# Tile 0 of a two-MLP kernel: half-width elementwise steps, bank-by-bank waits, and weight remainders split by groups on GpSimd

## What is computed

```python
w = exp(weight - max(weight)); w = w / (sum(w) + 1e-9)
x = sum over k of w[head, k] * x_pad[:, s + k, :]       # (2, 4096, 192)
x = x.reshape(8192, 192)
h = x @ w_in1;  g = h * clip(h + 3, 0, 6) / 6;  x = g @ w_out1      # 192 -> 2048 -> 192
h = x @ w_in2;  g = where(h > 0, h, exp(min(h, 0)) - 1)
out = g @ w_out2
```

## Time and profile before

| | us |
|---|---|
| median of 3 executions | 1120.57 (1120.43 to 1121.04) |
| profiled execution, its own time | 1120.58 |
| its span | 1118.7 |
| PE busy | 1113.0 (99% of the span), 9736 matmuls |
| DVE busy | 901.3 |
| ACT busy | 633.6 |
| POOL busy | 39.2, 36 instructions |

### The profile page before, as it was taken

One profiled execution on the slowest core, in us unless ns is written; L12 is line 12 of the kernel. 1 busy time (PEld: TensorE's weight loads), 2 busy tenths in 40 slices (PEclk: granted clock), 3 DMA queues, 4 the chain that ended last, 5 costly groups with the idle time before them and its releaser, 6 DMA issues.

```text
span 1118.7 us, 24069 instructions
## 1 busy us (share of the span) xinstructions
PE 1113.0 (99%) x9736; PEld 1014.5 (91%) x9736; DVE 901.3 (81%) x964; ACT 633.6 (57%) x685; POOL 39.2 (4%) x36
## 2 busy tenths in 40 slices
PE   9999999999999999999999999999999999999998
PEld 7999999999999999999999999999999999999997
DVE  8897887878888788787878878788787887876776
ACT  7765646556555554655555555465555655546544
POOL 3422000000000000000000000000000000000000
PEclk9999999999999999999999999999999999999999
DMA  4310010100101001010010100001000010000000
GB/s 158 117 59 10 1 34 0 33 0 0 33 0 33 0 0 33 0 33 0 0 33 0 33 0 1 32 0 33 0 24 9 0 33 0 9 5 11 6 2 29
DMA packets 10664, 22.48 MB, mean 20 GB/s; under 512 B 1424, under 2 KB 1424, under 8 KB 10640
## 3 DMA queue, kind: packets, MB, share of 16 engines
q1 hardware_dynamic: 10496, 22.12, 6.1%
q10 hardware_dynamic: 144, 0.01, 0.0%
HBM read 15.83 MB, written 6.29 MB: 20 GB/s over the span
## 4 chain that ended last, share of the span: by engine, by line
PE 98%; DVE 1%; DMA 0%; issue 0%; ACT 0%; DVEq 0%
PE h_ps L695 31%; PE acc_a L709 31%; PE acc_b L717 21%; PE h_ps L702 15%; DVE conv_a L466 0%; DMA taps<-tap_w 0%; PE h_ps L725 0%; DVE hidden L528 0%; PE acc_a L783 0%; PE acc_a L757 0%; PE acc_b L765 0%; PE acc_b L759 0%; PE acc_b L777 0%; PE acc_a L764 0%; PE acc_a L758 0%
## 5 line engine op out<-in xcount | busy, mean ns | idle before, releaser
L353 ACT CAST g_hi<-hidden 128x1024 fp32r<-128x1024 f32 x255 | 268.8, 1054 | 351.7 <-DVE hidden L533 238.2
L537 DVE TENSOR_TENSOR g_lo<-hidden,g_hi 128x1024 fp32r<-128x1024 f32 x255 | 312.9, 1227 | 127.7 <-ACT g_hi L353 127.7
L695 PE MATMUL h_ps<-in_hi_a,win_hi_a 64*128 64x512 f32 x1012 | 390.7, 386 | 0.0
L709 PE MATMUL acc_a<-g_hi,wout_hi_a 64*128 64x512 f32 x1012 | 390.7, 386 | 0.0
L695 PE MATMUL h_ps<-in_hi_a,win_lo_a 64*128 64x512 f32 x1012 | 390.6, 386 | 0.0
L709 PE MATMUL acc_a<-g_hi,wout_lo_a 64*128 64x512 f32 x1012 | 390.6, 386 | 0.0
L695 PE MATMUL h_ps<-in_lo_a,win_hi_a 64*128 64x512 f32 x1012 | 390.6, 386 | 0.0
L717 PE MATMUL acc_b<-g_hi,wout_b 64*128 64x512 f32 x1012 | 350.3, 386 | 0.0
L709 PE MATMUL acc_a<-g_lo,wout_hi_a 64*128 64x512 f32 x1012 | 310.1, 386 | 0.0
L717 PE MATMUL acc_b<-g_lo,wout_b 64*128 64x512 f32 x1012 | 310.0, 386 | 0.0
L528 DVE SCALAR_TENSOR_TENSOR hidden<-hidden,h_ps 128x1024 f32<-128x1024 f32 x128 | 156.3, 1221 | 59.0 <-ACT hidden L343 58.8
(11 more groups left out here) (112 smaller groups left out, 1212.9 us busy)
## 6 DMA issues: line engine op xcount, KB each, us to landing
xwin_a<-x_win SPq DMA_DIRECT2D x16, 259.0 KB, 2.8
raw_in<-w_in SPq DMA_DIRECT2D x8, 512.0 KB, 3.6
out_t<-out_a SPq DMA_DIRECT2D x16, 256.0 KB, 2.9
xwin_b<-x_win SPq DMA_DIRECT2D x15, 259.0 KB, 2.9
raw_out<-w_out SPq DMA_DIRECT2D x8, 384.0 KB, 3.9
out_t<-out_b SPq DMA_DIRECT2D x16, 128.0 KB, 2.3
xnext_b<-x_win SPq DMA_DIRECT2D x1, 259.0 KB, 5.5
taps<-tap_w ACTq DMA_DIRECT2D x1, 7.0 KB, 2.6
```

What stands on the lines that cost most here:

```text
L353: nc.scalar.copy(g_hi[:, g % PARTS, :], hidden[:, g % 2, :]).then_inc(hi_ready, 1)
L537: nc.vector.tensor_tensor(g_lo[:, g % PARTS, :], hidden[:, g % 2, :], g_hi[:, g % PARTS, :].bitcast(F32), ALU.subtract).then_inc(lo_ready, 1)
L695: return nc.tensor.matmul(bank(g, c), w[HALVES[r], columns(g, c)], x[HALVES[r], :], start=start, stop=c == 0 and r == 1 and term == 2)
L709: return nc.tensor.matmul(acc_a[acc][:, :], w[HALVES[r], g * CPG + c, :], x[HALVES[r], g % PARTS, c * TOK:(c + 1) * TOK], start=g == 0 and ...
```

## The change

1. ACT makes the relu of groups 0 and 1 in two halves, one for each bank; the first signals the new `act_half`, the second `act_done`.
2. DVE multiplies these two groups in halves (`nonlinear_halves`), with the new `g_half` after the first and `g_ready` after the second. Tap 0 goes ahead of group 0, and the finish of the b rows of tile 1 between groups 0 and 1.
3. `first_product` (group 2) waits before bank 0 for `g_half` and before bank 1 for `g_ready`.
4. ACT now makes the high parts of groups 0 and 1 back to back, then casts the a half of piece 3, then the relu of group 2, then casts the b half of piece 3.
5. POOL makes the low parts of pieces 2 and 3 in parts of one group each. `w_split` then counts: 1 is `win_lo_b` of piece 1 (waits for `act_half` 1); 2 and 3 are `wout_lo_a` and `wout_b` of group 0 (`act_half` 2); 4 is `win_lo_a` of group 4, 5 is `wout_lo_a` of group 1, 6 is `win_lo_b` of group 4, 7 is `wout_b` of group 1, 8 and 9 are `win_lo_a` and `win_lo_b` of group 5 (all wait for `act_done` 3, the relu of group 2). 10 and 11 are piece 4 as before, `wout_lo_a` and `wout_b` of groups 2 and 3.
6. PE waits for the parts of its group, and SP for the last part of a piece, before the buffer is filled again.

```diff
+        SPLITS = ([(1, 1, None), (2, 0, 0), (2, 1, 0), (3, 0, 0), (2, 0, 1), (3, 1, 0), (2, 1, 1), (3, 0, 1), (3, 1, 1)]
+                  + [(n, half, None) for n in range(4, ALL_PIECES) for half in range(2)])
+        BY_GROUPS = (2, 3)
+
+        def split(eng, n, half, part=1):
...
-                eng.wait_ge(w_split, h - 2)
+                eng.wait_ge(w_split, SPLITS.index((n, half, part if n in BY_GROUPS else None)) + 1)
...
-            together = [0, 0, 0, 0, 0, 1, 1, 2, 3, 3, 4, 4, 5, 5, 6, 7]
-            for n in range(1, ALL_PIECES):
+            together = {4: (3, 3), 5: (4, 4), 6: (5, 5), 7: (6, 7)}
+            for n, half, part in SPLITS:
+                raw, hi, lo = piece_views(n)[half]
+                if part is not None:
+                    if piece(n)[1] == 0:
+                        c = slice(part * CPG * P, (part + 1) * CPG * P)
+                        raw, hi, lo = raw[:, c], hi[:, c], lo[:, c]
+                    else:
+                        c = slice(part * CPG, (part + 1) * CPG)
+                        raw, hi, lo = raw[:, c, :], hi[:, c, :], lo[:, c, :]
+                h = 2 * n + half
                 piece_loaded(pool, n)
...
+                pool.wait_ge(w_hi, h + 1)
+                if n == 1 or (n == 2 and part == 0):
+                    pool.wait_ge(act_half, n)
+                elif n in BY_GROUPS:
+                    pool.wait_ge(act_done, 3)
+                else:
+                    pool.wait_ge(act_done, (together[n][half] if n < 8 else max(h - 9, GROUPS)) + 1)
+                nc.gpsimd.tensor_tensor(lo, raw, hi.bitcast(F32), ALU.subtract).then_inc(w_split, 1)
...
-            nonlinear(0, 0, 0)
-            nonlinear(0, 0, 1)
+            for g in range(2):
+                act.wait_ge(h_ready, g + 1)
+                for c, done in enumerate((act_half, act_done)):
+                    cols = slice(c * TOK, (c + 1) * TOK)
+                    nc.scalar.activation(hidden[:, g, cols], h_ps[g][:, cols], ACT.Relu,
+                                         bias=three[:, 0:1]).then_inc(done, 1)
             high_part(0, 0)
-            high_weights(3)
             high_part(0, 1)
+            piece_loaded(act, 3)
+            for half, (raw, hi, lo) in enumerate(piece_views(3)):
+                if half == 1:
+                    nonlinear(0, 0, 2)
+                nc.scalar.copy(hi, raw).then_inc(w_hi, 1)
             for g in range(2, GROUPS):
-                nonlinear(0, 0, g)
+                if g > 2:
+                    nonlinear(0, 0, g)
...
+            def nonlinear_halves(g):
+                for c in range(CPG):
+                    v = hidden[:, g, c * TOK:(c + 1) * TOK]
+                    dve.wait_ge((act_half, act_done)[c], g + 1)
+                    nc.vector.scalar_tensor_tensor(out=v, in0=v, scalar=6.0, in1=h_ps[g][:, c * TOK:(c + 1) * TOK],
+                                                   op0=ALU.min, op1=ALU.mult).then_inc((g_half, g_ready)[c], 1)
...
+            dve.wait_ge(tap_chain, 5)
+            conv_tap_a(0)
+            nonlinear_halves(0)
             dve.wait_ge(rest_done, 2)
             nc.vector.scalar_tensor_tensor(out=conv_b[:, :], in0=xnext_b[:, TAPS - 1:TAPS - 1 + TOK],
...
-            dve.wait_ge(tap_chain, 5)
-
-            nonlinear(0, 0, 0)
-            conv_tap_a(0)
-            nonlinear(0, 0, 1)
+            nonlinear_halves(1)
...
             def in_weights(m, g, load, half):
-                if load and g % 2 == 0:
-                    split(pe, number(m, 0, g // 2), half)
+                if load and (g % 2 == 0 or number(m, 0, g // 2) in BY_GROUPS):
+                    split(pe, number(m, 0, g // 2), half, g % 2)
...
                 in_weights(m, g, load, 0)
-                pe.wait_ge(g_ready, base + g - 1)
                 for c in range(CPG):
+                    pe.wait_ge((g_half, g_ready)[c], base + g - 1)
                     in_whole(m, g, src, c)
```

More of the change, by code:

```diff
@@ L144, in build @@
         act_done = sem("act_done")
+        act_half = sem("act_half")
+        g_half = sem("g_half")
         expm1_done = sem("expm1_done")
@@ L186, in number @@
             return 2 * PIECES * m + ORDER.index((kind, k))
-        def split(eng, n, half):
+        SPLITS = ([(1, 1, None), (2, 0, 0), (2, 1, 0), (3, 0, 0), (2, 0, 1), (3, 1, 0), (2, 1, 1), (3, 0, 1), (3, 1, 1)]
+                  + [(n, half, None) for n in range(4, ALL_PIECES) for half in range(2)])
+        BY_GROUPS = (2, 3)
+        def split(eng, n, half, part=1):
             h = 2 * n + half
@@ L289, in _ @@
                                         channel_multiplier=1).then_inc(ident_set, 1)
-            together = [0, 0, 0, 0, 0, 1, 1, 2, 3, 3, 4, 4, 5, 5, 6, 7]
-            for n in range(1, ALL_PIECES):
-                piece_loaded(pool, n)
[L295 to L301, removed]
+            together = {4: (3, 3), 5: (4, 4), 6: (5, 5), 7: (6, 7)}
[9 more added lines that the diff above has]
+                h = 2 * n + half
+                piece_loaded(pool, n)
+                pool.wait_ge(w_hi, h + 1)
[6 more added lines that the diff above has]
+                nc.gpsimd.tensor_tensor(lo, raw, hi.bitcast(F32), ALU.subtract).then_inc(w_split, 1)
         @block.scalar
@@ L734, in in_weights @@
             def in_weights(m, g, load, half):
-                if load and g % 2 == 0:
-                    split(pe, number(m, 0, g // 2), half)
+                if load and (g % 2 == 0 or number(m, 0, g // 2) in BY_GROUPS):
+                    split(pe, number(m, 0, g // 2), half, g % 2)
             def out_weights(m, g, load, half):
-                if load and g % 2 == 0:
-                    split(pe, number(m, 1, g // 2), half)
+                if load and (g % 2 == 0 or number(m, 1, g // 2) in BY_GROUPS):
+                    split(pe, number(m, 1, g // 2), half, g % 2)
             def first_product(m, base, g, src, load):
                 in_weights(m, g, load, 0)
-                pe.wait_ge(g_ready, base + g - 1)
                 for c in range(CPG):
+                    pe.wait_ge((g_half, g_ready)[c], base + g - 1)
                     in_whole(m, g, src, c)
@@ L939, in _ @@
             pair(1, "first")
-            pe.wait_ge(w_split, 2 * ALL_PIECES - 3)
+            pe.wait_ge(w_split, len(SPLITS))
             with nc.Fori(2, TILES - 1, engines=[mybir.EngineType.PE], hint_back_edge=True) as i:
```

## The result

The changed kernel has a median of 1122.39 us (1121.94 to 1123.42, 22 runs), the kernel before 1120.82 beside it (1120.36 to 1121.50, 22 runs). The ratio is 1.0015, with a 95% interval of 1.0009 to 1.0021: slower by 1.57 us, less than the 0.2% (2.24 us) by which the chances were set, but clear of noise with so many runs. The profiled execution took 1121.98 us, its span is 1120.2.

A forecast was written before the change was run, and what follows sets the result against it. PE's entry into its gapless stretch at 26.40 was taken to bound the kernel; -0.13 + 0.57 + 0.17 + 0.34 = +0.95 on 1120.58 gave 1121.5 us, range 1120.2 to 1122.6.

The forecast's parts named there:

- What bounds the kernel: PE is busy without gaps from 26.40 to 1107.00, so only its entry into that stretch moves the total.
- The gain: Tile 0: low part of group 0 ends at 18.40 instead of 18.53, so PE gains 0.13 us (bounds 0 to 0.25).
- (a): PE's first matmul of group 2, at 15.33, waited for DVE and could start at 14.85: 0.48 us lost.
- Turns of POOL and DVE: DVE steps with two SBUF operands and POOL remainders exclude each other and alternate, first asker first; low part 1.09 after release.
- Losses of rounds 4 and 5: PE waits for POOL's late count 7 (0.57), count 10 (0.17) and count 11 (0.34 us).
- the restarts: PE restarting after a stall can cost 0.07 more each, a bound of up to +1.2 us in total.
- The tie: POOL's count 9 at 24.44 against DVE's tap 2 at 24.50, given to POOL, ending at 25.18.
- rival 1: The near tie at 24.5 goes to DVE, PE starts round 5 at 28.2: +1.8, 1122.4 us; chance 0.20.
- the change touches tile 0 alone: The edit acts only in tile 0, so only PE before 26.40 matters; at most about 0.5 us to gain.
- Rival 2: POOL is in time as waiting DVE cannot step between back-to-back POOL parts: 1120.4, or 1120.0 with more gain; chance 0.25.
- Rival 4: The change does nothing: relu halves cost what multiply halves bring, POOL in time, 1120.6 us; chance 0.06.
- rival 3: Longer slide: piece 5 (round 6) late too, count 11 ending after 29.9; 1123.5 us or more; chance 0.04.

The follow-up runs named there:

- run 3: Changed kernel with DVE's taps 1 and 2 of tile 1's a rows moved from behind groups 2 and 3 to groups 4 and 5; 1123.59 us, ratio 1.0025.
- 9: Kernel before the change plus two real one-column copies on ACT in its idle time at the start; 1121.14 us, ratio 1.0002.
- 10: run 5's kernel plus two real one-column copies on ACT in its idle time at the start; 1120.58 us, ratio 0.9996.
- run 8: run 5's kernel with ACT's two relus whole and DVE's multiply of group 1 whole; 1121.26 us, ratio 1.0004.
- run 5: Changed kernel with POOL's piece 2 parts for group 1 ahead of piece 3, batch started behind group 0's high part; 1121.10 us, ratio 1.0001.
- run 2: Kernel before the change with only POOL's split by groups and its new waits, no halves; 1122.23 us, ratio 1.0013.
- 1: Changed kernel with the halves and ACT's new order, but POOL making whole pieces with its old waits; 1121.89 us, ratio 1.0009.
- 6: Kernel before the change with 4 empty instructions on ACT at the start; 1120.76 us, ratio 1.0000.

## Why the prediction was right, point by point

- **What bounds the kernel:** right for 1.10 of the 1.53 us found, which came from PE's entry into the gapless stretch; wrong for the other 0.43, which arose inside that stretch (below). The total was 1122.39, in the range, the forecast (1121.5) 0.9 short. Of this, 0.25 is the kernel before itself, whose median was 1120.57 in 3 executions and 1120.82 in 22; 0.15 is tile 0 (1.10 where +0.95 was forecast) and 0.43 the late Exp; the last 0.06 stays open.
- **The gain:** forecast 0.13 by the low part of group 0, measured 0.07 at round 4. The prices of the halves held: 1.27 for two relu halves (1.26), 1.28 for two on DVE (1.29). The steps behind it came as worked out, with 0.24 for this execution's start: group 2 at 14.61 (14.85 forecast), round 3 at 17.07 (17.31), the low part of group 0 at 16.96 (17.19) for 1.22. That (a) would turn into a wait at L809 was right: the lead of 0.38 at round 3 falls to 0.07.
- **Turns of POOL and DVE:** right, with their prices: 0.60 for 256 columns after a tap (0.61), 1.08 for a low part (1.09), 0.32 for the 128-column part that no row had shown (0.33). Count 7 ended at 23.57 (23.54 after the shift). The page "SBUF — State Buffer" of the Trainium skill, on its engine ports, calls this an exclusive lock; all runs agree, above all run 3, where taking one two-operand step away shortened two POOL parts from 1.18 and 1.44 to 0.74 and 0.46.
- **Losses of rounds 4 and 5:** forecast 0.57 + 0.17 = 0.74 up to round 5's start and 0.34 in round 5; measured 0.71 (5.03 less the 4.32 of before) and 0.46 (4.77 less 4.31), 0.09 more together. With the 0.24 added, the waits ended within 0.05 of the forecast: the first at 23.95 (23.90), round 5's start at 27.06 (27.01), the last at 28.74 (28.71). Most of what is missing are the restarts, which cost 0.08 each (28.50 to the next matmul is 0.31) and which I had left out of the sum and put in the bounds. The tie went as I had it; rival 1, at 1122.4, met the total by chance and not by its mechanism.
- **The rest of the 0.9:** the late Exp, 0.43. The step of the prediction that failed is "the change touches tile 0 alone", and with it that no wait of another engine reaches PE behind 26.40: the change also makes ACT's stream two instructions longer, and that is felt at a fetch of instructions 1050 us later (runs 9 and 10).
- **Rival 2** (POOL in time) fell by DVE's stepping in between back-to-back parts. The prediction also put a shared pair under this rival, which is another mechanism: shared, both sides would slow down together, while the rows show waits that end 0.32 to 1.16 after the other side's end. **Rival 4** (no effect) fell with the gaps in rounds 4 and 5; **rival 3** did not come about: count 11 ended at 28.35, not after 29.9.

## What to carry to other kernels

Two engines that exclude each other are scheduled by who asks first, so a plan for one is a plan for both: write down for each part when it is wanted, start the batch from an event that only the intended side is ready for (run 8), and put the most urgent part first (run 5); splitting into smaller parts alone cost 1.45 us (run 2). A gain ahead of a wait (here 0.48 at group 2) is worth only what the next wait behind it leaves. When nearly all runs of a family of kernels differ by a few tenths that tile 0 does not explain, compare the starts of the rounds over the whole span: one jump far from the edit can come from the program's length, as here.

## What was not expected of the hardware

- An ACT instruction was 1.1 to 1.4 us late where a fetch on queue 14 fell right ahead of it. This cost 0.24 to 0.62 in the seven kernels that had it, and nothing where two instructions more or less put the fetch ahead of an idle stretch. How the fetch holds ACT up is not shown.
- Queue 14 is not ACT's alone. Its fetches near 1069 move with the number of ACT's instructions (685, 687, 689), and not with those of DVE or POOL. But another, at 80 to 84 us in the kernels with 40 instructions on POOL, stands at 97 to 99 us in those with 36 (before, 1, 6 and 9). No record names the engine.
- Empty instructions on ACT (4, 16, 40) did not move its fetches and are in no record.
- The busy time of weight loads says nothing of pace: it is 1014.5 us before and 1105.8 after, and between 918 and 1107 in the other kernels, at the same 9736 loads and 4.31 us a round.
- The start of the first matmuls shifts by up to 1.1 us between profiled executions (last pair of group 1 from 14.28 to 15.38), which is more than the whole effect of most edits here.
